# Six expert blocks of batches 0 and 1 computed between the attention tiles of batches 2 and 3

## What is computed

```
attention: scores = q k^T / sqrt(64) per head; only the 32 largest scores of a row are kept;
           softmax over them; times v          (4 batches, 8 heads, 576 tokens, 64 per head)
MoE:       logits = x @ w_gate (8 experts), local = sigmoid(x @ w_local), per token s in order:
           e[s] = argmax(logits[s]) if s == 0 or local[s] < 0.5 else e[s-1]
           out[s] = softmax(logits[s])[e] * (relu(x[s] @ w1[e]) @ w2[e])      (512 -> 1024 -> 512)
mixer:     u = x + real(fft(fft(x, tokens), channels)); layer norm; u + relu(un @ w_ch1) @ w_ch2
```

## Time and profile before

| | us |
|---|---|
| median of 3 runs (1560.2 to 1563.28) | 1562.87 |
| the profiled execution | 1560.65 |
| its span, first to last instruction | 1558.8 |
| TensorE busy, share of the span | 1417.2, 91% |
| VectorE busy, share of the span | 1075.7, 69% |
| ScalarE and GpSimd busy | 604.3 and 624.9 |
| mean granted clock of TensorE, of full speed | 0.926 |

### The profile page before, as it was taken

How to read it: one execution, slowest core, us unless ns; L and a number is a source line. 1 busy time by engine, 2 the same in 40 slices (tenths; PEclk the granted TensorE clock), 3 DMA queues, 4 the chain that set the end, 5 groups by cost and what they waited for, 6 DMA issues and landing times. The chain is left out here.

```text
span 1558.8 us, 24264 instructions
## 1 busy us (share of the span) xinstructions
PE 1417.2 (91%) x8476; PEld 1214.2 (78%) x8476; DVE 1075.7 (69%) x2133; ACT 604.3 (39%) x1469; POOL 624.9 (40%) x502
## 2 busy tenths in 40 slices
PE   6898898989888998985999999967999999999998
PEld 4777777777677777774899999953777789999987
DVE  7999999999999999998455555546646422422222
ACT  4555455555455555541444444413322221321111
POOL 4666666666866666660244444422202100000000
PEclk9889898898999988986899999975999999999999
DMA  9110111111011011102017356442322011411111
GB/s 324 34 33 28 29 32 32 33 32 28 14 31 32 25 32 32 69 1 75 32 59 260 132 193 234 160 153 89 128 75 71 31 41 65 138 41 41 41 41 61
DMA packets 67146, 117.01 MB, mean 75 GB/s; under 512 B 27283, under 2 KB 27412, under 8 KB 67042
## 3 DMA queue, kind: packets, MB, share of 16 engines
q1 hardware_dynamic: 57306, 87.19, 16.9%
q0 software_dynamic: 8928, 27.00, 4.9%
q10 hardware_dynamic: 808, 1.48, 0.3%
HBM read 87.33 MB, written 30.42 MB: 76 GB/s over the span
## 5 line engine op out<-in xcount | busy, mean ns | idle before, releaser
L332 POOL TENSOR_SCALAR keep<-s_sb,top 128x576 f32<-128x576 f32 x142 | 244.4, 1721 | 224.2 <-DVE top L356 224.2
L356 DVE MAX8 top<-w_sb 128x8 f32<-128x576 f32 x432 | 304.0, 744 | 0.0
L227 PEld LDWEIGHTS ps_o<-v_sb,eT 128*128 128x128 f32 (+1 forms) x1440 | 202.0, 206 | 37.7 <-issue 26.3
L227 PE MATMUL ps_o<-v_sb,eT 128*128 128x74 f32 (+3 forms) x1440 | 225.4, 298 | 0.0
L1367 DVE SCALAR_TENSOR_TENSOR h_lo<-ps_ch,h_hi 128x384 fp32r<-128x384 f32 x96 | 53.4, 556 | 242.1 <-ACT h_hi L1218 242.0
L358 DVE MATCH_REPLACE8 w_sb<-top,w_sb 128x576 f32<-128x576 f32 x288 | 211.2, 739 | 0.0
L336 POOL TENSOR_TENSOR e_sb<-e_sb,keep 128x576 f32<-128x576 f32 x142 | 200.0, 1408 | 21.8 <-POOL keep L332 0.6
L199 PE MATMUL ps_t<-ident,e_sb 128*128 128x128 f32 x576 | 107.0, 315 | 84.4 <-POOL e_sb L336 78.7
L210 PE MATMUL ps_o<-ident 128*128 128x128 f32 x1152 | 180.5, 309 | 0.0
L210 PEld LDWEIGHTS ps_o<-ident 128*128 128x128 f32 x1152 | 167.1, 223 | 1.9 <-ACT rows L301 0.7
L783 PEld LDWEIGHTS ps_h<-bxT,w 128*128 128x128 f32 x1408 | 162.4, 194 | 3.4 <-issue 1.6
(11 more groups left out here) (214 smaller groups left out, 2409.9 us busy)
## 6 DMA issues: line engine op xcount, KB each, us to landing
w<-in_w SPq DMA_DIRECT2D x18, 2048.0 KB, 13.5
stage<-in_w_ch SPq DMA_DIRECT2D x16, 512.0 KB, 3.5
q_sb<-in_q SPq DMA_DIRECT2D x16, 288.0 KB, 2.8
vT<-in_vt SPq DMA_DIRECT2D x16, 288.0 KB, 3.1
x_d<-rows SPq DMA_DIRECT2D x18, 256.0 KB, 2.4
u<-u_d SPq DMA_DIRECT2D x18, 256.0 KB, 2.9
x_d<-u POOLq DMA_DIRECT2D x18, 256.0 KB, 2.6
u<-x_d SPq DMA_DIRECT2D x18, 256.0 KB, 2.8
```

The lines of the kernel that those rows point to most:

```text
L227: mm = pe.matmul(ps_o[k % 2][:, lo:hi], eT[k % NT_][0:n, c, :], v_sb[b][0:n, c, lo:hi], start=(c == 0), stop=(c == KC))
L332: pool.tensor_scalar(keep[t % 2][:, :], s_sb[t % NS][:, :], top[t % NS][:, TOPK - 1:TOPK], None, ALU.is_ge).then_inc(s_keep, 1)
L356: dve.max(eight, src).then_inc(s_top, 1)
```

## The change

The tokens of batches 0 and 1 are routed on their own while VectorE works on the pairs 38 to 43: `early_routing` is a generator, and up to two of its operations are issued behind each of the 14 operations of a pair. TensorE's small products for it (`HOPS`) stand in the iterations 74 to 79. All tokens of batches 0 and 1 are sorted by expert, with an expert's full blocks ahead of all partly filled ones, and the first six (`NA`) blocks are run inside `attention`: their work is cut into 105 units (`UNITS`: "x" turns the rows, "h" is four matmuls with w1, "y" one matmul with w2, in plain fp32 with 512 columns). 96 units stand in the iterations 83 to 140, one or two in each, and nine behind the last tile. From iteration 83 on `keep_clock` is left out. The units need two PSUM banks, which the scores give up: a pair's scores are now made in two halves in two iterations, and ScalarE copies 288 columns at a time. ScalarE also moves the units' results out of PSUM and issues the loads of the weights, GpSimd gathers the rows and scatters the results, and waits for the last scatter at the end of `attention`. SyncE stores the rows of x of batches 0 and 1 in the middle and no longer loads weights at the start. The second routing takes the tokens of batches 2 and 3 together with those that the six blocks left; the steps that find a token's expert (`choice`) now run on 9 tiles instead of 18. `experts` is as before, with `SURE` 12 instead of 18.

The diff, cut:

```diff
+HT = NT // 2
+NA = 6
+FAR = float(1 << 19)
...
+def choice(dve, step, hop, env, r, h, oh):
+
+    lg, cst, ident = env["lg"], env["cst"], env["ident"]
+    ts = slice(HT * h, HT * h + HT)
+    im8, later = cst[:, C_IM8:C_IM8 + E], cst[:, C_LATER + HT * h:C_LATER + HT * h + HT]
+    dve.wait_ge(env["s_cst"], 32)
+    dve.scalar_tensor_tensor(r["keeps"][:, :], lg[:, ts, E], 0.0, later, ALU.is_ge, ALU.mult).then_inc(r["s_go"], 1)
...
+    yield from hop(0)
+    dve.wait_ge(r["s_back"], T_KEEPS)
+    yield from step(dve.tensor_copy(r["keepT"][:, :], r["ps_keep"]))
...
+    MIDDLE = NTILE // 2
+    ROUTE, NORM = MIDDLE // 2 + 2, MIDDLE + 3
+    HOPS = [(MIDDLE + n, at) for n, at in ((2, 2), (3, 2), (4, 1), (4, 2), (5, 2), (7, 2))]
+    AWAIT = [(ROUTE + n, at) for n, at in ((0, 9), (1, 0), (1, 7), (1, 10), (2, 0), (3, 4))]
...
-        ps_s = [pb(f"ps_s{n}", [P, 2, 512]) for n in range(2)]
+        ps_s = [pb(f"ps_s{n}", [P, 512]) for n in range(2)]
+        ps_a = [pb(f"ps_a{n}", [P, 512]) for n in range(2)]
...
+        UNITS = [("x", 0, 0)] + [("none", 0, 0)] * 3
+        for j in range(NA):
+            UNITS += [("h", j, m) for m in range(NF)] + [("y", j, m) for m in range(NF // 2)]
+            UNITS += [("x", j + 1, 0)] if j + 1 < NA else []
+            UNITS += [("y", j, m) for m in range(NF // 2, NF)]
+        EARLY0, EARLY1, LATE = MIDDLE + 11, NTILE - 3, 9
+
+        def units_at(t):
+            main = len(UNITS) - LATE
+            if t < EARLY1:
+                at = lambda x: max(main * (x - EARLY0) // (EARLY1 - EARLY0), 0)
+                return UNITS[at(t):at(t + 1)]
+            first = main + 3 * (t - NTILE - 2)
+            return UNITS[first:first + 3] if t >= NTILE + 2 else []
...
-            for c in range(2):
-                load_w1(sp, env, (0, E - 1)[c], c)
-                load_w2(sp, env, (0, E - 1)[c], c)
...
+            store_x(0)
+            load_pair(NPAIR // 4 + 1, 0)
+            load_pair(NPAIR // 4 + 1, 1)
+            with sp.Fori(NPAIR // 4 + 2, NPAIR // 2) as i:
+                for b in range(2):
+                    load_pair(i, b)
+            store_x(1)
...
-            for t in range(-LQ, NTILE + 2):
+            for t in range(-LQ, NTILE + 10):
...
+                if k + h > 0:
+                    pe.wait_ge(s_copy, 2 * k + 2 * h)
+                score(k, h).then_inc(s_qk, 1)
+                score(k + 1, h).then_inc(s_qk, 1)
...
+            def early_h(j, m, bank):
+                if m == 0:
+                    pe.wait_ge(a["s_xT"], j + 1)
+                    pe.wait_ge(a["s_w1"][j % 2], 16 * (j // 2) + 16)
+                if m == NF // 2:
+                    if j > 0:
+                        pe.wait_ge(a["s_yv"], j)
+                    else:
+                        pe.wait_ge(a["s_idx"], IDX_GATE)
+                for k in range(KC):
+                    mm = pe.matmul(bank[:, (m % KC) * P:(m % KC + 1) * P], env["w1"][j % 2][:, k, m * P:(m + 1) * P],
+                                   a["xT"][:, k, :], start=(k == 0), stop=(k == KC - 1))
+                if m % (NF // 2) == NF // 2 - 1:
+                    mm.then_inc(a["s_h1"], 1)
...
+                mm = pe.matmul(bank[:, :], a["h"][:, m, :], env["w2"][j % 2][:, m, :], start=(m == 0), stop=(m == NF - 1))
+                if m == NF - 1:
+                    mm.then_inc(a["s_y"], 1)
...
+                for n, unit in enumerate(units_at(t)):
+                    if n % 3 == at:
+                        early(*unit)
+
             def body(t):
                 if live(t):
                     if t == 0:
                         pe.wait_ge(env["s_ident"], 1)
                     turn(t)
-                    keep_clock(t)
-                if live(t + LQ) and (t + LQ) % 2 == 0:
-                    scores(t + LQ)
+                    if t < EARLY0:
+                        keep_clock(t)
+                between(t, 0)
+                k = t + LQ
+                if live(k):
+                    scores(k - k % 2, k % 2)
+                between(t, 1)
                 if live(t - 1):
                     values(t - 1)
+                between(t, 2)
...
+                if t == EARLY0 - 4:
+                    act.wait_ge(a["s_idx"], IDX_E)
+                    for j in range(2):
+                        early_w1(j)
+                        early_w2(j)
+                for unit in units_at(t):
+                    early(*unit)
...
+                    act.activation(a["h"][:, half * NF // 2:(half + 1) * NF // 2, :].rearrange("p m q -> p (m q)"),
+                                   ps_a[(j + half) % 2][:, :], ACT.Relu).then_inc(a["s_h"], 1)
+                    if half == 1:
+                        early_w1(j + 2)
...
+                    act.activation(a["y"][:, :], ps_a[j % 2][:, :], ACT.Copy, scale=a["gcol"][:, j:j + 1]).then_inc(a["s_yv"], 1)
+                    early_w2(j + 2)
...
+            def scatter(j):
+                pool.wait_ge(a["s_yv"], j + 1)
+                if j == 0:
+                    pool.wait_ge(a["s_idx"], IDX_S)
+                for n, dst in enumerate((env["y_d"], env["r_d"])):
+                    pool.indirect_dma_start(out=dst, out_offset=bass.IndirectOffsetOnAxis(ap=a["sidx"][:, n, j:j + 1], axis=0),
+                                            in_=a["y"][:, :], in_offset=None,
+                                            bounds_check=B * S - 1, oob_is_err=False).then_inc(a["s_yo"], 16)
...
+                    if t == unit_tile(("y", j, NF - 1)) + 4:
+                        scatter(j)
...
+            pool.wait_ge(a["s_yo"], 32 * NA)
...
+            def step(ins):
+                made[0] += 1
+                at = made[0]
+                ins.then_inc(s_rt, 1)
+                yield
+                dve.wait_ge(s_rt, at)
+
+            def hop(n):
+                while now[0] < AWAIT[n]:
+                    yield
...
+                yield from step(dve.tensor_scalar(a["left"][:, :], a["blk"][:, :], float(NA), None, ALU.is_ge))
+                yield from step(dve.tensor_tensor(env["oh"][:, :, 0:HT], a["oh"][:, :, :],
+                                                  a["left"][:, None, :].broadcast_to([P, E, HT]), ALU.mult))
+                yield from step(dve.tensor_scalar(env["place"][:, E, 0:HT], a["left"][:, :], -FAR, FAR, ALU.mult, ALU.add))
...
+                    now[0] = (c, n)
+                    if c >= ROUTE:
+                        next(routing, None)
+                        next(routing, None)
...
-            then(logits(slice(0, TPP), 0, 1))
...
-        SURE = NT
+        SURE = NT - NA
```

More of the change, by code:

```diff
@@ L88, in attention, with unit_tile @@
         s_norm = [sem(f"s_norm{b}") for b in range(2)]
+        s_rt = sem("s_rt")
+        r, a = choice_buffers(nc, ctx, "_a", ps_a), early_buffers(nc, ctx, env)
         block = ctx.enter_context(nc.Block(no_gpsimd_drain=True))
         LAST = NTILE - TPP
+        cst = env["cst"]
+        ones, below = cst[:, C_ONE:C_ONE + P], cst[:, C_UP:C_UP + P]
+        NF = F // P
+        UNITS = [("x", 0, 0)] + [("none", 0, 0)] * 3
[11 more added lines that the diff above has]
+            return UNITS[first:first + 3] if t >= NTILE + 2 else []
+        def unit_tile(unit):
+            return next(t for t in range(EARLY0, NTILE + 8) if unit in units_at(t))
         @block.sync
```

519 lines of the change are left out of this document (369 added, 150 removed).

## The result

The changed kernel takes 1578.95 us (median) against 1561.53 us for the kernel before in the same comparison: ratio 1.0103, 95% interval 1.0076 to 1.0131. It is slower by 1%. (The ratio leaves out one execution of the changed kernel, which took 1624.95 us at a granted clock of 0.83 where the others have 0.92 to 0.93.) The forecast was 1515.7 us, faster by 3%, and its range of 1503 to 1540 does not hold the result.

A forecast was written before the change was run, and what follows sets the result against it. VectorE bounds attention, TensorE the expert stage. -78.1 + 17.0 + 3 + 3 + 9 - 1 = -47.1 us from the profiled 1560.65 gives 1513.6, plus 2.2 for the median: 1515.7 us, range 1503 to 1540.

The forecast's parts named there:

- Removed: six blocks: Expert stage: 16 blocks instead of 22, at 13.01 us each, save 78.1 us.
- fewer blocks are saved: Rival, expert stage: two-part routing leaves more partly filled blocks, 17 or 18 instead of 16; 1529 or 1542 us, chance 0.04.
- Missing blocks' branches: Behind the last expert block: branches for nine missing blocks instead of three cost +0 us, end +1.
- Added on VectorE: Pairs 38 to 43: 69 added routing operations, the 58 small ones at mean 0.226 us, cost +17.0 us, ends 15 and 19.
- waits (+3): Pairs 38 to 43: VectorE waits at six places for small TensorE products, one late at pair 40's start; ends 0 and 8.
- TensorE lateness and the split: Attention: split scores shorten the copies' lead, so low-clock stretches cause a handful of short stalls, +3 us, ends 0 and 12.
- TensorE between the tiles: Iterations 83 to 140: without dummies but with units TensorE needs 4.44 of 4.83 us a tile, so VectorE stays the bound.
- both TensorE rivals: Units' iterations: TensorE becomes the bound, 1539 us, chance 0.2; or TensorE stays at 1.2 GHz, 1686 us, chance 0.03.
- The end of attention: Behind the last pair: nine units, scaling and scatter delay the second routing's start from 719.84 to 729.0, +9 us.
- Second routing: Second routing: a dozen operations on half the width save 1 us.

The follow-up runs named there:

- the repaired table: The change with only the first routing's scan mask corrected, a zero at every 9th place instead of every 18th: 1531.47 us, ratio 0.9824.
- the late split: Scores split only from tile 78 on, added to the change with corrected scan mask, later GpSimd scatter wait and nested missing blocks: 1512.32 us, ratio 0.9688.
- the split's own run: The kernel before, with only the scores made in two halves and copied 288 columns at a time: 1568.68 us, ratio 1.0056.
- The last two versions: The change with corrected mask, later scatter wait, nested missing blocks, scores split from tile 78: 1512.32 us; then also all 105 units in iterations 83 to 144: 1506.97 us.
- the version with the moved wait: The change with corrected scan mask, and GpSimd's wait for the last early scatter moved into the second routing: 1523.49 us, ratio 0.9761.

## Why the prediction was wrong

**Removed: six blocks (-78.1).** This step failed, and it alone turned the sign. The price of a block was right (13.02 us against 13.01, and 78.3 for six with the repaired table). The count of 16 was not: it rested on what the first routing is meant to compute and not on what its scan computes with the table it reads. The change made 20, and the step measured -25.9 us. The rival "fewer blocks are saved" named the right outcome by another mechanism (more partly filled blocks), and was sized at 17 or 18 blocks with a chance of 0.04, because the count agreed with the 22 of the kernel before. That agreement said nothing of the new sort, which is other code. The step's cue was in the text of the change: a scan over `HT * E` places with a table built for `NT * E`.

**Missing blocks' branches (+0, end +1).** Too low for the version that was forecast. With 9 missing blocks it is 8.3 us to the mixer's first load, because TensorE walks until 14.9 us behind its last product (994.2 to 1009.1) and the scatter covers only 6.8 of the time. In the change, with 5 missing, it is +1.0, and GpSimd's, not TensorE's. The 6.8 us of the earlier trace rows held 3 such branches under cover and could not tell what nine would do; the end of the range should not have been +1.

**Added on VectorE (+17.0) and waits (+3).** Close, in part by luck. The pairs 38 to 43 take 82.8 us instead of 58.7, so +24.1, of which 4.5 are the two waits above and 19.6 the operations, just beyond the end of 19. All of it lies in four pairs, not six: 15.8, 14.5, 17.3 and 15.9 us. What the mean of 0.226 us missed is in the last section. The waits are not the forecast ones: at the pair 40's start, where it had a late product, VectorE waits for nothing in the change (in four of the other versions 1.9 to 2.2 us). The 1.9 us are for a product in the pair 39, and the 2.6 us for a score copy in front of the pair 42, behind ScalarE's first four weight loads. The forecast had put the issue of the loads at nothing, under cover of the copies' lead; in every other version that leaves the dummies out 1.9 to 3.3 us stand there too.

**TensorE lateness and the split (+3, ends 0 and 12).** The mechanism, half clock and a shorter lead, is seen, but not where the units run: there VectorE never waits in the change, and all but two stalls of the other versions that leave the dummies out there lie ahead of the pair 38 or behind ScalarE's first loads. The change's profiled execution has none of them, only the 2.6 us just told. For the median the size stays open between the 1.3 us that the late split gives back and the 8.1 us of the split's own run.

**TensorE between the tiles (4.44 of 4.83 us).** Right, if a little fuller. 230.6 of 240 us busy is 96% where 92% was forecast, the clock is 0.97, and VectorE never waits there; both TensorE rivals fell. The unit of w2 takes 7.03/8 = 0.88 us against 0.95.

**The end of attention (+9).** Low by 4. Up to the end of the last scaling the working holds to 0.1 us: 747.31 - 727.57 = 19.7, forecast 723.0 - 703.38 = 19.6. Then the change takes 9.3 us to the next stage where the earlier trace rows had 6.0. That row was measured with no 2 MB load beside the scatter, and in the tail ScalarE issues two, 8.3 and 1.5 us ahead of it; the run that holds them back ends the stage 3.5 us sooner behind its scatter. The rest, 0.4 us, is VectorE's start behind GpSimd.

**Second routing (-1).** +0.2. The narrower operations take 0.23 us instead of 0.31, and VectorE's chain ends 0.4 us sooner (21.1 us long instead of 21.5), less than the 1 us forecast; the first block then takes 0.6 us longer to its scaling.

With 16 blocks the kernel takes 1531.5 us, in the profiled execution 17.6 more than the sum allowed: 10.3 behind the last block, 4.5 in the tail, 1.7 up to the last pair, 1.3 in routing, less 0.2 of the blocks. The last two versions undo the first two of these and land at 1512.3 and 1507.0.

## What to carry to other kernels

When a change saves work by a count that the program makes at run time, follow the count through the new code with the tables it really reads; that the result stays right proves nothing when leftovers have a second path. Price what is walked past as well as what is run, and on every engine: here five skipped blocks stayed under a scatter, and nine cost 8 us that nesting the conditions took away. And a stage that waits for a scatter at its end should have no large load issued beside it (2.8 us became 6.8), or should leave the wait to the first reader.

## What the hardware showed

**A half clock that lasts while TensorE never idles.** In the profiled execution of the version with the moved wait, TensorE dropped to a granted clock of 0.50 (1.2 GHz) at 251.8 us, during an idle 1.72 us, and stayed there until 292.8 us, with no idle time from 260 us on; VectorE waited 3.8 us at most for a copy and 11.0 us in all:

```profile
240.00:260.00 20.00, 16.84 (x91) 13.53 (x90) 20.00 (x42) 8.88 (x28) 13.21 (x9) 0.80 0.10 24
260.00:280.00 20.00, 20.00 (x82) 16.13 (x81) 17.23 (x38) 7.87 (x24) 11.35 (x8) 0.50 0.12 39
280.00:300.00 20.00, 20.00 (x104) 16.65 (x104) 13.77 (x29) 9.32 (x32) 10.72 (x7) 0.68 0.01 2
```

The forecast took a handful of short stalls, and counted for the full clock that TensorE has it where it never idles. Here over 30 us without idle time did not bring it back, and the pairs 26 to 28 took 9 us longer.

**VectorE's small operations end with GpSimd's.** Five operations of the first routing, on 8 to 96 elements of a partition, took about 1.0 to 1.5 us instead of 0.2, and each ended within 0.1 us of a two-operand operation of GpSimd. Two of them in the change's timeline, with GpSimd's:

```profile
406.24 1.40 POOL L662 TENSOR_TENSOR e_sb<-e_sb,keep 128x576 f32<-128x576 f32 x1
406.64 1.03 DVE L739 TENSOR_SCALAR early_cnt<-early_cnt 128x16 int32<-128x16 int32 x1
...
410.50 1.40 POOL L662 TENSOR_TENSOR e_sb<-e_sb,keep 128x576 f32<-128x576 f32 x1
410.53 1.38 DVE L746 SCALAR_TENSOR_TENSOR early_move<-early_move,early_full 128x8 f32<-128x8 f32 x1
```

1.38 is the remainder of GpSimd's 1.40, and 1.03 that of the one begun 0.4 earlier. The five add some 4.8 us. Without them the operations would have taken 14.8 us, so they are why the sum came out above the forecast, whose mean was taken from the old routing, where GpSimd is mostly at rest (3.7 of 21.9 us busy). Not every small operation is held: five others that began beside such an operation of GpSimd took 0.13 to 0.23 us, two TENSOR_REDUCE, a RECIPROCAL, and two with an input in PSUM. The Trainium skill ("GPSIMD Engine Reference", Specifications) says that GpSimd and VectorE share SBUF interfaces and contend when VectorE has two SBUF inputs or runs in a two-port mode. The trace agrees for the second pair of rows, and for the five that were not held, none of which has two SBUF inputs. The first pair has a single input, as have two of the five that were held, and only such a mode could bring them under the rule. No run here tried this by itself.
